# Attention, routed experts and a dense layer: other order around the expert changes, quarter products and leading products of zeros

## The reference

```python
# attention over a state of 32 rows, both ways; B, H, S, Ns, D = 8, 8, 512, 32, 64
scores = scale * x @ state.T;  a  = softmax(scores);   xread = a @ state
scores2 = scale * state @ x.T; a2 = softmax(scores2);  sread = a2 @ x
x = concat([xread, sread]) -> 4352 rows of 512
# one expert of eight for each row (512 x 1024, 1024 x 512)
logits = norm(x) @ norm(expert_emb).T / tau
e = argmax(logits);  gate = softmax(logits)[e]
x = gate * (relu(x @ w1[e]) @ w2[e])
# dense layer, 512 x 2048 x 512
out = (s * relu(x @ w_in) ** 2 + b) @ w_out
```

## Time and profile before

| | us |
|---|---|
| median of three runs | 1391.1 (1390.35 to 1391.83) |
| the profiled execution | 1393.17 |
| its span in the profile | 1391.1 |
| attention, about | 0 to 125 |
| routed tiles, about | 125 to 618 |
| dense layer, about | 618 to 1391 |

### The profile page before, as it was taken

The page is one execution under the profiler, slowest core; times in us unless marked ns, Lnnn a source line. Parts: engine busy times, 40 slices in busy tenths (PEclk is TensorE's granted clock), DMA queues, the critical chain, the costliest instruction groups (busy, mean ns, idle before and its releaser), DMA issues.

```text
span 1391.1 us, 23074 instructions
## 1 busy us (share of the span) xinstructions
PE 1345.2 (97%) x6908; PEld 1105.3 (79%) x6909; DVE 645.1 (46%) x1648; ACT 506.7 (36%) x951; POOL 192.6 (14%) x341
## 2 busy tenths in 40 slices
PE   7998899999999999999999999999999999999996
PEld 5776688877788778779888888888888888888884
DVE  5898546666645664757323223232232332322322
ACT  4885335545434643544222222222222222222221
POOL 2236322221222122200001001000010010100101
PEclk9999999999999999999999999999999999999998
DMA  8755313553512451240100001001010010100000
GB/s 252 224 145 193 115 57 103 180 184 108 184 49 68 149 185 49 71 170 9 48 0 31 32 0 62 0 15 47 0 62 0 0 62 0 62 0 0 31 0 31
DMA packets 71938, 103.61 MB, mean 74 GB/s; under 512 B 40424, under 2 KB 41048, under 8 KB 70624
## 3 DMA queue, kind: packets, MB, share of 16 engines
q1 hardware_dynamic: 57824, 72.16, 15.8%
q0 software_dynamic: 8448, 20.40, 4.4%
q10 hardware_dynamic: 5632, 10.60, 2.0%
HBM read 71.81 MB, written 31.34 MB: 74 GB/s over the span
## 4 chain that ended last, share of the span: by engine, by line
PE 81%; DVE 7%; issue 4%; DMA 2%; DVEq 2%; POOL 1%; ACT 1%; ACTq 0%; POOLq 0%; SPq 0%
PE bank_a L1570 26%; PE bank_n L1589 14%; PE bank_tt L1589 12%; PE bank_a L1492 11%; PE bank_n L1525 10%; DMA xg<-x_tok,g_idx 2%; PE bank_tt L1505 1%; PE bank_n L1423 1%; DVEq L363 1%; POOL slot_tab L497 1%; PE bank_tt L1294 1%; PE bank_a L1275 1%; DVE w_in_lo L1044 1%; DVEq L366 1%; PE bank_l L1556 1%
## 5 line engine op out<-in xcount | busy, mean ns | idle before, releaser
L1212 DVE TENSOR_TENSOR sq<-rel 128x512 f32<-128x512 f32 (+1 forms) x144 | 95.4, 663 | 478.4 <-ACT rel L817 478.4
L817 ACT ACTIVATE rel<-bank_a 128x512 f32<-128x512 f32 (+1 forms) x144 | 82.8, 575 | 534.9 <-PE bank_a L1570 534.9
L1570 PE MATMUL bank_a<-y_hi,w_in_hi 128*128 128x512 f32 (+1 forms) x576 | 218.1, 379 | 1.5 <-DVE y_lo L1204 1.4
L1570 PE MATMUL bank_a<-y_hi,w_in_lo 128*128 128x512 f32 (+1 forms) x576 | 217.6, 378 | 0.0
L1570 PE MATMUL bank_a<-y_lo,w_in_hi 128*128 128x512 f32 (+1 forms) x576 | 217.6, 378 | 0.0
L582 POOL DMA_INDIRECT out_rows<-w_raw,out_id x34 | 32.9, 968 | 714.5 <-DVE w_raw L1223 652.1
L1570 PEld LDWEIGHTS bank_a<-y_hi,w_in_hi 128*128 128x128 f32 x576 | 108.4, 188 | 23.0 <-DVE y_lo L1204 1.8
L1570 PEld LDWEIGHTS bank_a<-y_lo,w_in_hi 128*128 128x128 f32 x576 | 108.4, 188 | 20.6 <-issue 0.2
L1570 PEld LDWEIGHTS bank_a<-y_hi,w_in_lo 128*128 128x128 f32 x576 | 108.4, 188 | 19.9
L1525 PE MATMUL bank_n<-w_hi,hid_hi 128*128 128x512 f32 x296 | 115.5, 390 | 1.5 <-DVE hid_lo L1069 1.5
L1525 PE MATMUL bank_n<-w_hi,hid_lo 128*128 128x512 f32 x296 | 115.4, 390 | 0.0
(11 more groups left out here) (237 smaller groups left out, 2136.3 us busy)
## 6 DMA issues: line engine op xcount, KB each, us to landing
w_raw<-in_moe_w SPq DMA_DIRECT2D x16, 2048.0 KB, 10.6
moe_tok<-yg ACTq DMA_DIRECT2D x38, 272.0 KB, 2.1
x_tok<-x_rows SPq DMA_DIRECT2D x8, 1088.0 KB
y_rows<-moe_tok SPq DMA_DIRECT2D x8, 1088.0 KB, 5.3
x_m<-in_x SPq DMA_DIRECT2D x7, 1024.0 KB, 9.4
win_raw<-in_moe_w_in SPq DMA_DIRECT2D x8, 512.0 KB, 10.7
w_raw<-in_moe_w_out SPq DMA_DIRECT2D x1, 4096.0 KB, 16.2
slot_tab<-w_lo SPq DMA_DIRECT2D x2, 1152.0 KB, 6.6
```

What stands on the lines that cost most here:

```text
L817: nc.scalar.activation(rel[:, k, 0:cols], ps_g[k][:, 0:cols], ACT.Relu).then_inc(rel_ready, 1)
L1212: nc.vector.tensor_tensor(sq[:, 0:cols], rel[:, k, 0:cols], rel[:, k, 0:cols], ALU.mult).then_inc(sq_ready, 1)
L1570: last = nc.tensor.matmul(ps_g[n % 2][:, 0:cols], w[:, wc], a[:, c, 0:cols], start=(c == 0 and w is w_in_hi and a is y_hi), stop=(c == DC ...
```

## The change

- TensorE does four products (`IDLE = 4`) of a zeroed tile (320 columns) before its first transpose.
- In batch 0 the other states are turned behind the scores, the embedding products come behind the state read, and ScalarE's first two evacuations of batch 1 behind the exponential; VectorE's `evac_st` calls move behind the subtraction.
- Both halves of the turned token weights are evacuated by ScalarE.
- `state_read` works per head: 32 states by 64 columns on a quarter of the array's columns, twice as many products of half the columns.
- ScalarE and VectorE load a tile's registers at its beginning; ScalarE's `store` goes behind `next_w2`; VectorE's gate is cut in two, with `next_w2` between.
- The table has one word more (the tile ahead of the last); the loop's last turn is written out without the work for a tile that does not exist.

```diff
@@ TensorE
+            pe.wait_ge(hot_zero, 1)
+            zeros = lg_all[:].rearrange("p b t e -> p (b t e)")
+            for _ in range(IDLE):
+                nc.tensor.matmul(bank_n2[0][:, 0:B * COLS * E], zeros[:, 0:P], zeros, start=True, stop=True)
             pe.wait_ge(const_ready, 3)
...
             for i in range(B):
                 if i >= 1:
                     scores(i)
+                if i >= 1:
+                    turn_a1(i - 1)
+                    turn_rows(i - 1)
+                turn_scores(i)
                 if i == 0:
                     pe.wait_ge(diag_ready, 16 * (P // NS))
                     for k in range(1, B // 2):
                         st_transpose(k)
-                else:
-                    turn_a1(i - 1)
-                    turn_rows(i - 1)
-                turn_scores(i)
                 turn_e2(i)
-                if i == 0:
-                    embed_states()
-                else:
+                if i >= 1:
                     row_logits(i - 1)
...
                 state_read(i)
+                if i == 0:
+                    embed_states()
@@ state_read
-                        for par in range(2):
-                            p = slice(HP * par, HP * par + HP)
-                            j = 2 * jj + par
-                            last = nc.tensor.matmul(bank_r[p, jj * P:(jj + 1) * P], a2_n[:, t, jj * P + HP * par:jj * P + HP * par + HP],
-                                                    x_m[bb % 3][:, t, j * P:(j + 1) * P], start=(t == 0), stop=(t == TPB - 1))
+                        for q in range(P // NS):
+                            p = slice(NS * q, NS * q + NS)
+                            c = (q % 2) * DH
+                            h = jj * (P // NS) + q
+                            last = nc.tensor.matmul(bank_r[p, jj * P + c:jj * P + c + DH], a2_n[:, t, jj * P + NS * q:jj * P + NS * q + NS],
+                                                    x_m[bb % 3][:, t, h * DH:(h + 1) * DH], start=(t == 0), stop=(t == TPB - 1))
@@ TensorE, tiles
-            with pe.Fori(2, last_g) as g:
+            prev = tile_ahead_of_last(pe)
+            with pe.Fori(2, prev) as g:
                 tile(g)
+            turn_hidden(prev)
+            up(last_g)
+            down(prev)
             turn_hidden(last_g)
@@ ScalarE
             def a1_evac(bb):
-                act.wait_ge(a1_tr, 2 * bb + 1)
...
+                for jj in range(2):
+                    act.wait_ge(a1_tr, 2 * bb + jj + 1)
+                    if jj == 0 and bb >= 1:
+                        act.wait_ge(xread_done, TPB * bb)
+                    nc.scalar.activation(a1_t[:, jj, :], bank_a[jj][:], ACT.Copy).then_inc(a1_ready, 1)
...
                 a2_evac(i)
-                if i + 1 < B:
+                if 1 <= i < B - 1:
                     for j in range(2):
                         x_evac(i + 1, j)
                 act.wait_ge(sh_done, i + 1)
                 nc.scalar.activation(e1[:], e1[:], ACT.Exp, scale=-1.0).then_inc(e1_done, 1)
+                if i == 0:
+                    for j in range(2):
+                        x_evac(1, j)
...
             def tile(g):
+                e, changes = experts(g)
+                e_next, changes_next = experts(g + 1)
+                row = rows_of(act, g)
                 hidden(g + 1)
                 x_hi(g + 2)
                 gate_square(g + 3)
-                next_w1(g + 1)
+                next_w1(e_next, changes_next)
                 gate_soft(g + 1)
                 result(g)
                 hidden_hi(g + 1)
-                store(g)
-                next_w2(g)
+                next_w2(e, changes, e_next)
+                store(g, row)
...
+            hidden(last)
+            gate_soft(last)
+            result(prev)
+            hidden_hi(last)
+            e_a, c_a = experts(prev)
+            e_b, _ = experts(last)
+            next_w2(e_a, c_a, e_b)
+            store(prev)
@@ VectorE
-                if i >= 1:
-                    a1_evac(i - 1)
-                else:
+                if i == 0:
                     embed_turned()
-                    for k in range(1, B // 2):
-                        evac_st(k)
...
                     .then_inc(sh_done, 1)
+                if i == 0:
+                    for k in range(1, B // 2):
+                        evac_st(k)
...
+            def experts(g):
+                return expert_of(dve, g), changes_after(dve, g)
...
+            def gate_norm(g):
...
+                rsqrt_rounds(gate_link, gc[:, 4:5], gc[:, 5:6], gc[:, 0:1], 1)
+            def gate_root(g):
...
+                rsqrt_rounds(gate_link, gc[:, 4:5], gc[:, 5:6], gc[:, 0:1], 2)
...
             def tile(g):
+                e, changes = experts(g)
+                e_next, changes_next = experts(g + 1)
                 x_lo(g + 2)
                 gate_logits(g + 3)
-                next_w1(g + 1)
+                next_w1(e_next, changes_next)
                 gate_final(g + 1)
                 hidden_lo(g + 1)
-                gate_scale(g + 2)
-                next_w2(g)
-
-            with dve.Fori(2, last) as g:
+                gate_norm(g + 2)
+                dve.sem_inc(norm_turn, 1)
+                next_w2(e, changes, e_next)
+                gate_root(g + 2)
+
+            with dve.Fori(2, prev) as g:
                 tile(g)
+            gate_final(last)
+            hidden_lo(last)
+            e_a, c_a = experts(prev)
+            e_b, _ = experts(last)
+            next_w2(e_a, c_a, e_b)
...
+            tab_step(nc.vector.tensor_scalar(tab_o[:, 3 * NSLOT + 1:3 * NSLOT + 2], acc[:, src, 0, 2 * E - 1:2 * E], -2.0, None, ALU.add))
@@ GpSimd
-            with pool.Fori(2, last) as g:
+            with pool.Fori(2, prev) as g:
                 gather(g + 3)
                 result_ids(g)
+            result_ids(prev)
             result_ids(last)
```

More of the change, by code:

```diff
@@ L39, in attention_moe_ffn @@
     SOON_ST = 2
+    IDLE = 4
     COLS = TPB + 1
@@ L99, in attention_moe_ffn @@
         gi = sb(top, "gi", [P, 2], i32)
-        used = sum(-(-n // 32) * 32 for n in (4 * P, 4 * P, 2 * P, 2 * P, 4 * PAIRS * E, 4 * (3 * NSLOT + 1), 4 * IDW, 4, 4 * NSLOT, 4 * NSLOT,
+        used = sum(-(-n // 32) * 32 for n in (4 * P, 4 * P, 2 * P, 2 * P, 4 * PAIRS * E, 4 * (3 * NSLOT + 2), 4 * IDW, 4, 4 * NSLOT, 4 * NSLOT,
                                               4, 4, 4, 4 * TROWS, 4 * E, 4 * E, 32, 8))
@@ L443, in _ @@
             sp.sem_inc(load_turn, 1)
-            sp.wait_ge(gate_sq, last + 3)
+            sp.wait_ge(gate_sq, last + 2)
             sp.sem_inc(load_turn, 1)
@@ L701, in win_hi, with next_w1 @@
                 nc.scalar.activation(w_in_hi[:, ds(e * SLOT, SLOT)], win_raw[:], ACT.Copy).then_inc(win_hi_done, 1)
-            def next_w1(g):
-                e = expert_of(act, g)
-                with act.If(changes_after(act, g) > 0):
+            def experts(g):
+                return expert_of(act, g), changes_after(act, g)
+            def next_w1(e, changes):
+                with act.If(changes > 0):
                     act.wait_ge(w1_loaded, 16 * e + 32)
@@ L709, in next_w1, with next_w2 @@
                         nc.scalar.activation(w1_hi[:, c], w_raw[:, c], ACT.Copy).then_inc(w1_hi_done, 1)
-            def next_w2(g):
-                e = expert_of(act, g)
-                with act.If(changes_after(act, g) > 0):
+            def next_w2(e, changes, e_next):
+                with act.If(changes > 0):
                     act.wait_ge(w2_loaded, 16 * e + 32)
@@ L742, in result, with store @@
                 nc.scalar.activation(yg[:, 0:D], ps_y0 if starts(g) else ps_y, ACT.Copy, scale=gate_s[:, ds(g, 1)]).then_inc(yg_ready, 1)
-            def store(g):
+            def store(g, row=None):
+                row = rows_of(act, g) if row is None else row
                 act.wait_ge(yg_ready, g + 1)
                 act.wait_ge(yid_done, g + 2)
-                act.dma_start(moe_tok[ds(rows_of(act, g), P), :], yg[:]).then_inc(moe_stored, 16)
+                act.dma_start(moe_tok[ds(row, P), :], yg[:]).then_inc(moe_stored, 16)
             x_hi(0)
@@ L787, in tile @@
                 hidden_hi(g + 1)
-                store(g)
-                next_w2(g)
-            with act.Fori(2, last) as g:
+                next_w2(e, changes, e_next)
+                store(g, row)
+            with act.Fori(2, prev) as g:
                 tile(g)
+            hidden(last)
[6 more added lines that the diff above has]
+            store(prev)
             def wout_hi(n):
@@ L848, in emb_link, with rsqrt_seed, rsqrt_rounds @@
                 dve.wait_ge(emb_step, n_emb[0])
-            def rsqrt_steps(link, y, t, n2, iy, it):
+            def rsqrt_seed(link, n2, iy, it):
                 link(nc.vector.tensor_single_scalar(it, n2.bitcast(i32), 1, ALU.arith_shift_right))
                 link(nc.vector.tensor_scalar(iy, it, -1.0, RSQRT_SEED, ALU.mult, ALU.add))
-                for _ in range(3):
```

(9 more changed lines are left out.)

58 lines of the change are left out of this document (34 added, 24 removed).

## The result

| | before | after |
|---|---|---|
| median of four runs each, timed side by side | 1391.5 us (1390.4 to 1392.2) | 1412.2 us (1410.6 to 1414.1) |
| ratio, 95% interval | | 1.015 [1.0132, 1.0168] |
| span of the profiled execution | 1391.1 | 1412.1 |
| mean granted TensorE clock | 0.993 | 0.981 |

The change costs 20.7 us. The forecast was 1397.5 with a range of 1384 to 1405: slower was right, the size was not.

What follows compares the result with a forecast made beforehand. In attention batches TensorE (12.36 of 13 us) and VectorE (12.32) both bound; the dense stage was taken as equal. Attention -6.5, last tile -2.4, expert changes +15.4 sum to +6.5 us: 1397.5 us, range 1384 to 1405.

Steps and rivals of the forecast that it cites:

- +2.2 x 7 = +15.4 us: Seven expert changes: xg_lo starts 2.2 us later at each, behind gate steps, branch and four loads; bounds 11 to 17.5 us.
- the loads run ahead: Rival at expert changes: VectorE's sequencer fetches registers while a gate step waits, xg_lo 1.1 us earlier, 1374 in all; chance 0.12.
- VectorE's queue cannot run ahead of them: Expert changes: each moved gate step waits for the one before, so branch and four loads (2.9 us) follow, ahead of xg_lo.
- Every sign that the text named for "right": Half-length score product by 10 us, state read near 1.05, batches 12.4, four loads before xg_lo, changes 16.3 us, no dense-stage gap.
- 6.5 us earlier: Attention stage: start, first batch's order and steady batches together end it 6.5 us earlier, between 0 and 9.
- The zeros: Start: products of zeros raise TensorE's clock by about 8 us; 2.5 us gained, between 0.9 lost and 3.2 gained.
- The steady batch: Attention: quarters save 0.90 us, ScalarE's second turned half costs 0.42, so a batch goes from 12.89 to 12.4 us.
- it starts that much earlier: End of attention: GpSimd's slot writes and row fetch, up to the landing, start earlier by the attention's 6.5 us.
- lie beside these writes: End of attention: the second last-tile load (0.7 us) and added table step (0.2 us) run alongside GpSimd's slot writes.
- The quarters do not pack: Rival in attention: state read stays 1.9 us or more, ScalarE's added half is paid, attention gains nothing, 1404; chance 0.20.
- -2.4: Last tile and hand-over to the dense stage: y_lo starts earlier, dense products follow directly; 2.4 us less, between 1.8 and 2.8.
- A balance: Rival: xg_lo later by 1 us or less and attention gives its full 9 us, 1385 to 1393; chance 0.14.

Runs made afterwards that it cites:

- the second execution: The changed kernel, unchanged, timed and profiled again beside its variants on one chip: 1412.0 us, 1.0154 of the kernel before.
- the second profile of the kernel before: The kernel before, unchanged, run again for a trace on the same chip as changed versions: 1391.6 us, ratio 1.000.

## Why the prediction was right or wrong

- **The expert changes, "+2.2 x 7 = +15.4 us": the mechanism was right, and so nearly was the size.** 13.5 us, 1.9 a change. xg_lo began at 243.4, 14.3 us behind the up products where it had been 12.3; the forecast had 14.5. That the sequencer does not fetch registers while a gate step is waited for held; the rival *the loads run ahead* (0.12) is refuted where it was asked, but it is true one piece further on: under the long low halves, which nobody's next step waits for in turn, the loads do run ahead (the version with the gate in one piece). The trace of the kernel before has this too: two loads run from 239.3 to 240.4, under low halves that last until 241.3. The step "VectorE's queue cannot run ahead of them" named the right condition.
- **The step that failed is one that was left out: the clock behind the longer gap stood in the sum at nothing.** The sum went from the longer wait straight to the total, with every later product at its old duration. The text had both levels of the clock in its hands, used them for the start, and made the gap three microseconds long without asking what the clock does behind it. It fell seven times out of seven: +10.4 us, of the 14.7 by which the forecast was short. With it the sum would have been 1408; most of the rest is the attention. Every sign that the text named for "right" came, from the half score product to four loads ahead of xg_lo; none of them looked at how long TensorE's products take behind the gap.
- **The attention, "6.5 us earlier": 1.0 by the fifth up products in the profiled execution, 3.3 in the second.** Its parts came out well: the last batch's scores start 6.1 us earlier in the second execution. The zeros: full speed by 8.6 us, batch 1's scores 1.7 us earlier with them than without. The steady batch: 12.4 forecast, 12.5 measured; the quarters gave 0.7 us a batch (forecast 0.9), and ScalarE's second half cost 0.3 (13.2 with the old state read against 12.9 before; forecast 0.42). Wrong was "it starts that much earlier": GpSimd does start the slot writes 4.2 us earlier, but then waits for ScalarE's squares of the first rows before it can fetch again, and for the ranks of batches 6 and 7. Both stand behind the first row fetch, which took 6.7 us, and TensorE's part of it ran at the lower clock. Taking the wait for the ranks away brought only 1.2 us. The second last-tile load did not "lie beside these writes": with the five others it stands between a gate and xg_lo, and costs 1.0 us. A gain of 5.3 us in the last batch's scores was worth 1.6 at the end.
- **The quarters do not pack** (0.20) fell: 64 products in 1.10 us. The rule of the Trainium skill, TensorEngine Tiling (Array Packing), section Instruction Overhead, gives each product an overhead of about 60 cycles; added to the columns, that makes (60 + 64) / (60 + 128) of 1.97, an estimate of 1.3 us. So the rule spoke for a smaller gain than the forecast's, and not for a state read of 1.9 us or more; the trace has 1.10, below this estimate too. The 64 products of 8 columns in two halves took 2.04 us, 32 ns each, and do show a floor, whether of the product or of the operand that each of them loads.
- **The last tile, "-2.4":** -1.9. The gap of 1.39 us in the earlier trace rows is gone.
- **A balance** (0.14) did not come: it needed xg_lo late by 1 us or less, and it was late by 2.0.
- **The range** ended at 1405 since it was built of the quarters' case. No case had the clock in it, so none reached 1412.

## What to carry to other kernels

A register load on an engine's queue is free under long work that no one waits for step by step, and costs its full time (0.7 us on VectorE, 0.5 on TensorE) behind a chain of linked small steps or behind a semaphore wait. The same holds ahead of a loop as in it. So look at what stands in front of a load (and, on the engine that waits, load ahead of the wait), not at how many there are. When a wait on TensorE grows, price its products behind the gap at the lower clock as well: here three microseconds of gap cost another 1.5 in the tile after it.
An edit that shortens one stage is worth what the next queue in line lets through: ask for it there (here GpSimd's fifteen writes), before adding it up.

## What the runs showed of the hardware

- At the expert changes the granted clock fell at idle gaps of TensorE of 3.06 to 3.17 us at seven of seven, in two executions; at gaps of 1.65 us at two of seven; at gaps up to 0.4 us, in the other versions, at none. A single gap of 1.39 us, ahead of the dense stage, did not bring it down. It came back after 3.4 or 6.8 us in which TensorE was working at the lower level. In the start-up a run of shorter waits was enough once: low from 120.5 to 124.0 us in the second profile of the kernel before, behind waits of 0.43 and 1.16 us.
- Which changes cost 14.5 and which 13.2 us behind them was nearly the same in two executions.
- With products of zeros from 1.33 us on, the first score half (8.6 to 9.1 us) took 1.08 us in every profile that had them, while in the kernel before the one at 9.3 us took 1.98 us and the one at 13.9 us as long; there the products are at full speed by 18 us. In the one profile of the changed order without zeros they are by 13.8 us. In the profiled execution of the changed kernel the granted clock was low from 24.8 us on, behind a start-up with short waits (24.80 above: eight products in 3.93 us); in the second execution it was not.
- 64 products of 64 columns on four quarters of the array's columns take 1.10 us, 17 ns each, where 32 of 128 columns on two halves take 1.97: with four side by side the time halves with the columns.
